# Moving the mask block and the small statistics inside one SBUF arena, and an earlier wait for the load of the spatial bias

## The reference, cut to what matters

```python
# attention, 8 heads of 64, window of 128 keys and 4 sink keys
scores = scale * q @ k.T;  scores = where(keep, scores, -1e9)
a = exp(scores - max(scores));  x = (a / (sum(a) + 1e-9)) @ v
# gated mixer
h = relu(x @ w_in);  u, v = h[..., :512], h[..., 512:]
v_n = (v - mean(v)) / sqrt(var(v) + 1e-6)
v_s = einsum('ts,bsd->btd', w_spatial, v_n) + b_spatial[None, :, None]
y = (u * v_s) @ w_out
# token mixer and channel mixer
h = relu(y.transpose(0, 2, 1) @ w_tok1) @ w_tok2
u = y + h.transpose(0, 2, 1)
out = u + relu(u @ w_ch1) @ w_ch2
```

## Time and profile before

| | us |
|---|---|
| three runs | 523.14, 522.19, 522.09 |
| median | 522.19 |
| the profiled execution, its own time | 523.14 |
| its span on the profile | 521.4 |
| PE busy | 498.1 (96% of the span) |
| DVE, ACT, POOL busy | 217.3, 151.7, 178.5 |

### The profile page before, as it was taken

The page is one execution under the profiler, slowest core; times in us unless marked ns, Lnnn a source line. Parts: engine busy times, 40 slices in busy tenths (PEclk is TensorE's granted clock), DMA queues, the critical chain, the costliest instruction groups (busy, mean ns, idle before and its releaser), DMA issues.

```text
span 521.4 us, 7223 instructions
## 1 busy us (share of the span) xinstructions
PE 498.1 (96%) x2712; PEld 442.9 (85%) x2712; DVE 217.3 (42%) x535; ACT 151.7 (29%) x315; POOL 178.5 (34%) x192
## 2 busy tenths in 40 slices
PE   2589999999999999999999999999999999999997
PEld 1578899999999989999888899888888888888885
DVE  4577777587567434755221232112121121211212
ACT  3246656466555342111221122110101101001010
POOL 5566645375343278900406912950000000000000
PEclk9999999999999999999999999999999999999999
DMA  7524332433220134300201410410001000010002
GB/s 264 163 89 156 104 96 77 126 119 105 84 82 0 47 121 127 92 15 1 75 1 61 137 47 6 136 40 1 0 19 63 0 1 0 18 64 1 0 1 80
DMA packets 19478, 34.18 MB, mean 66 GB/s; under 512 B 2288, under 2 KB 4848, under 8 KB 19440
## 3 DMA queue, kind: packets, MB, share of 16 engines
q1 hardware_dynamic: 19008, 33.55, 20.3%
q10 hardware_dynamic: 432, 0.13, 0.1%
HBM read 30.53 MB, written 3.15 MB: 65 GB/s over the span
## 4 chain that ended last, share of the span: by engine, by line
PE 89%; DVE 4%; issue 2%; DMA 1%; POOL 1%; ACT 1%; DVEq 0%; ACTq 0%; SPq 0%
PE bank L933 23%; PE bank L935 23%; PE bank L934 23%; PE bank L1006 7%; PE bank L972 3%; PE bank L948 2%; PE bank L949 2%; PE bank L1014 1%; PE bank L988 1%; PE bank L1166 1%; DVE q_st L751 1%; DMA mask_scratch<-key 1%; PE bank L1164 1%; DVE masked L760 1%; DMA stage<-w_sp 1%
## 5 line engine op out<-in xcount | busy, mean ns | idle before, releaser
L922 DVE SCALAR_TENSOR_TENSOR hch_lo<-bank,hch_hi 128x512 fp32r<-128x512 f32 x36 | 24.9, 692 | 153.8 <-ACT hch_hi L696 153.8
L696 ACT ACTIVATE hch_hi<-bank 128x512 fp32r<-128x512 f32 x36 | 21.5, 598 | 169.0 <-PE bank L935 169.0
L588 ACT ACTIVATE probs<-masked,small 128x288 f32<-128x288 f32 (+1 forms) x96 | 49.1, 512 | 64.4 <-DVE small L760 64.2
L760 DVE CUSTOM_DVE_ANT_0 masked<-bank,masks 128x288 f32<-128x288 f32 (+1 forms) x96 | 40.9, 427 | 38.4 <-PE bank L949 32.7
L935 PE MATMUL bank<-up_hi,wc_lo 128*128 128x512 f32 x144 | 56.0, 389 | 0.0
L934 PE MATMUL bank<-up_lo,wc_hi 128*128 128x512 f32 x144 | 56.0, 389 | 0.0
L933 PE MATMUL bank<-hch_hi,wc_hi 128*128 128x512 f32 x144 | 56.0, 389 | 0.0
L934 PE MATMUL bank<-hch_lo,wc_hi 128*128 128x512 f32 x144 | 56.0, 389 | 0.0
L933 PE MATMUL bank<-up_hi,wc_hi 128*128 128x512 f32 x144 | 56.0, 389 | 0.0
L935 PE MATMUL bank<-hch_hi,wc_lo 128*128 128x512 f32 x144 | 56.0, 389 | 0.0
L948 PE MATMUL bank<-k_hi,q_st 128*128 128x288 f32 (+1 forms) x96 | 35.5, 372 | 18.2 <-DVE q_st L751 12.8
(11 more groups left out here) (120 smaller groups left out, 1067.2 us busy)
## 6 DMA issues: line engine op xcount, KB each, us to landing
k_raw<-kT SPq DMA_DIRECT2D x24, 256.0 KB, 3.1
q_raw<-qT SPq DMA_DIRECT2D x24, 256.0 KB, 2.7
stage<-w_c SPq DMA_DIRECT2D x24, 256.0 KB, 2.6
v_sl<-vL SPq DMA_DIRECT2D x12, 264.0 KB, 2.8
outT<-out_sb SPq DMA_DIRECT2D x12, 256.0 KB, 2.1
stage<-w_sp SPq DMA_DIRECT2D x12, 192.0 KB, 2.5
stage<-w_in SPq DMA_DIRECT2D x8, 256.0 KB, 3.6
stage<-w_out SPq DMA_DIRECT2D x4, 256.0 KB, 3.2
```

The source lines that it names most:

```text
L588: act.activation(probs[:, n % N_PROB, 0:w], masked[:, n % N_MASKED, 0:w], ACT.Exp, bias=least[:, n % 8:n % 8 + 1], scale=-1.0).then_inc(ex ...
L696: act.activation(hch_hi[:, u[2] % N_HCH, :], bank[:, :], ACT.Relu).then_inc(hi_ready, 1)
L760: dve.tensor_tensor_reduce(masked[:, n % N_MASKED, 0:w], score_bank[n % 2][:, 0:w], masks[:, m:m + w], 1.0, 3e38, ALU.add, ALU.min, least[ ...
L922: dve.scalar_tensor_tensor(out=hch_lo[:, f % N_HCH, :], in0=bank[:, :], scalar=0.0, in1=hch_hi[:, f % N_HCH, :], op0=ALU.max, op1=ALU.subt ...
```

## The change

The order inside the arena changes and one wait is replaced. The masks move from the front part of region A to its end, the small statistics to the end of the arena; `brow` now lies over the masks, 64 columns in, and so it needs the last masked head and no longer the last `x_lo`. Everything from `A_MASKED` to `A_X` starts 1,088 columns lower, everything from `B_X` to `E_IDR` 96 columns lower. An assertion that named offsets are multiples of 128 columns goes.

```diff
 A_VS = A_V + 3 * H * DV
-A_MASKS = A_VS + 2 * GV
-E_SMALL = A_MASKS + MASK_COLS
-A_MASKED = E_SMALL + 96
+A_MASKED = A_VS + 2 * GV
 A_PROBS = A_MASKED + N_MASKED * BAND
 ...
 A_X = A_CAT + P
-A_END = A_X + 2 * DM
+A_MASKS = A_X + 2 * DM
+A_END = A_MASKS + MASK_COLS
 B_X = A_END
 ...
 E_IDR = E_ID + P
-COLS = E_IDR + P
-
-assert all(at % P == 0 for at in (A_V, A_PROBS, A_PT, A_PTS, A_CAT, A_X, B_X, X_SLOT, B_WIN, C_VN, D_U, E_V, E_STAGE, E_ID))
+E_SMALL = E_IDR + P
+COLS = E_SMALL + 96
 ...
-A_BROW = A_CAT
+A_BROW = A_MASKS + 64
 ...
             for n in range(EARLY, EARLY + 3):
                 stage_in(n)
-            sp.wait_ge(x_lo_ready, TILES)
+            sp.wait_ge(masked_ready, N_HEAD)
             sp.dma_start(brow[:, :], b_sp).then_inc(s_brow, 16)
             for n in range(EARLY + 3, len(pieces)):
                 stage_in(n)
```

## The result

| | before | after |
|---|---|---|
| median of 6 runs each, us | 522.64 | 529.58 |
| lowest to highest | 522.09 to 523.81 | 527.68 to 531.05 |
| ratio after / before, 95% interval | | 1.0124 [1.0102, 1.0146] |
| profiled execution, span | 521.4 | 526.5 |

The change makes the kernel 1.2% slower, 5.3 to 7.6 us by the interval. The forecast was no change, at most 523.3. A ratio in this text is the one on record and not always the quotient of two medians: that of the change follows from the median of all 23 recorded runs of the changed kernel, 529.11 us.

A forecast was written before the change was run, and what follows sets the result against it. The prediction took PE as the bound, busy 498.1 of 521.4 us. Its three terms, 0 + 0 + 0, left the earlier median of 522.19 unchanged: 522.1 us, range 521.1 to 523.3.

The forecast's parts named there:

- Part 1, the wait: SP's bias load before the spatial products: goes out about 11.0 us earlier, but PE gains 0, lower end -0.31 us.
- rival (a): Entry to spatial products: PE does wait for the twelfth vn_lo, gain 0.31 us, total 521.9; chance 0.08.
- Part 2, the offsets: Operands of all engines at moved start addresses: no instruction gets longer or shorter, 0 us.
- So PE and DVE pay 0 here: PE products and DVE operations: durations at the four distances in the earlier trace look alike, so moved places cost 0.
- Part 3, transfers: Loads and stores touching moved rows: 0 us, with -0.1 and +0.1 as ends for the last store.
- (b): Start, DVE against POOL at L734: the race turns, DVE gains 1.02 us, total 521.2 or lower; chance 0.10.
- (c): Start, DVE mask chain L717 to L723: late index table loses a race with POOL, 1.1 to 1.4 us, 523.4; chance 0.10.

The follow-up runs named there:

- e5: The changed kernel with the old wait (12 times x_lo) put back, so only the places differ from the kernel before; 529.17 us, ratio 1.0115.
- e3: The kernel before with every buffer, region A too, 32 columns (128 bytes) higher; 523.05 us, ratio 1.0007.
- e2: The kernel before with B_X starting 32 columns (128 bytes) behind A_END, the assertion taken out; 530.41 us, ratio 1.0164.
- e4: The kernel before with 32 columns put in ahead of C_VN only, moving vn, y, w_c2 and the hidden layer; 525.42 us, ratio 1.0037.
- f1: The kernel before with `up` and `hch` products alternating in the mixer, B_X up 32 columns and D_U another 32; 526.96 us, ratio 1.0106.
- f0: The kernel before with `up` and `hch` products alternating one by one in the channel mixer, offsets unchanged; 522.46 us, ratio 0.9998.
- e9: The changed kernel with A_END rounded up by 32 columns; 522.14 us, ratio 0.9997.
- e7: The kernel before with 16 columns (64 bytes) put in ahead of B_X; 525.82 us, ratio 1.0064.
- e10: The kernel before with 48 columns (192 bytes) put in ahead of B_X; 528.2 us, ratio 1.0078.

## Why the prediction was wrong

**Part 1, the wait: right.** Its value was forecast as 0, and no run shows another: e1 (early wait, old offsets) gives 1.0019 [0.9999, 1.004], and e5 (late wait, new offsets) is as slow as the change. The steps came out as worked: bias load at 171.29 (said: near 172), the last vn_lo ahead of everything PE asks for (193.08; said 193.8), PE's start still 0.36 us behind ACT. The reading of vn_ready's value against the named releaser held, and rival (a) fell, most plainly by e5, where PE starts before the twelfth vn_lo has ended. The worked size, at most 0.31 us, was never paid out, since ACT's end decides in both kernels.

**Part 2, the offsets: wrong, and the step that failed is "So PE and DVE pay 0 here".** It put at 0 a term that the stages measure at 5.8 us. The sentence behind it dismissed "-1 and +1 cycle per product" as inside the rounding. What was measured is 5.5 ns for a product of 512 columns in w_out (226.9 to 232.4) and 2.7 ns for one of 384 (173.6 to 176.3), and 1,368 products stand in the four stages that grew. Three things were wrong in that step. First the variable: I compared an operand's place with a fixed grid. e3 shows that the place alone is of no account; e2 and e4 show that the distance between the operands counts. Second the resolution: the earlier trace rows has 10 ns steps (0.30 us), and an effect of 5 ns can't be seen in them. The earlier trace rows has single ns, but the length of a weight load is nearly blind to this effect: for the `up` products, which lose 6 ns each, its minimum, median and maximum are 187/188/188 before and 187/188/193 after. The view of one line has three digits, and it would have shown that the streams of 512 columns behind the attention are even to 3 ns (387/389/390, 389/389/389), a rhythm that had something to lose. Third the place: heads 92 and 93 in the earlier trace rows do happen to have distances 0 and 128 between q and k_lo, but they lie in the interleaved stage, where one such product stands between others. That no rhythm can build up there is my reading; the second token products of e4 and f1, which keep their length at distance 128 among short products, fit it. In the uniform stages, where PE has no slack at all, every product had distance 0. What never varies in the stretch at stake can't be bounded from another stretch, and the range should have carried the end instead of leaving it out.

**Part 3, transfers: about right, and small.** Stores land in 2.0 us in the median against 2.1. That fits in sign what the prediction took from the Trainium skill, page "DMA: Bandwidth & Descriptors", section "How a descriptor splits into AXI transactions". The other runs agree: the six profiles whose rows of `out_sb` start on a multiple of 256 bytes all show 2.0, and of the eight others seven show 2.1 and one (f0) 2.0. The staging loads of w_sp show nothing of the kind: 2.4 against 2.5 here, but 2.6 in e2, e3 and e5, which are aligned, and 2.4 in e1 and e9, which are not. None of it reached PE.

**The rivals on the start.** DVE's mask chain and the races with POOL, after:

```profile
7.15 0.35 DVE L719 SCALAR_TENSOR_TENSOR mask_scratch<-mask_scratch,small 128x128 f32<-128x128 f32 x1
7.53 1.24 DVE L721 TENSOR_TENSOR mask_scratch<-mask_scratch 128x128 f32<-128x128 f32 x1
8.80 0.31 DVE L706 TENSOR_SCALAR masks<-mask_scratch 128x128 f32<-128x128 f32 x1
...
15.29 1.39 DVE L732 TENSOR_TENSOR mask_scratch<-mask_scratch 128x128 f32<-128x128 f32 x1
```

The first race turned for the better (0.35 us for 1.43 in the earlier trace rows) and the one behind it for the worse (1.24 for 0.37); the third stayed lost. The first mask is ready 0.20 us earlier (8.80 + 0.31 = 9.11 against 8.59 + 0.72 = 9.31 before, by this line of the kernel before).

```profile
8.59 0.72 DVE L708 TENSOR_SCALAR masks<-mask_scratch 128x128 f32<-128x128 f32 x1
```

So (b) and (c) describe something real, but it is scatter between executions. e5 differs from the changed kernel only in SP's wait near 170 us, and yet its first race is lost again (1.35 us) and the second won (0.29). The kernel before and f0 are the same program up to the channel mixer, and the first spatial product starts at 195.3 us in one and 193.3 in the other; over the fourteen profiles it is anywhere from 193.3 to 198.1. So nothing here ascribes to the change the 0.7 us by which the changed kernel entered earlier. Rival (c), the slower one, named the wrong place: no rival priced PE's own stream.

**The size.** The sum over the stages, 5.8 us, lies inside the interval of the ratio (5.3 to 7.6 us). For e2 the interval is 6.6 to 10.6 us, and the same stages explain 5.8 of it; for e7 it is 2.0 to 4.7 us, and they explain 1.9. The rest is not explained; a later entry into the spatial products, which scatters, may be part of it.

## What to carry to other kernels

Where PE streams product after product without a hole, keep the start addresses of stationary and moving operand a multiple of 256 bytes apart, from one product to the next as well (e4's switches); when a layout is repacked, round each region's end, even if the assertion that says so looks like tidiness. Read the spread of a group's durations (387/389/390 against 390/394/405) and not only its mean, and multiply nanoseconds by the number of products before calling them rounding. A releaser named by a view is the last engine to touch a semaphore; the value in the code decides whether it was waited for.

## What the runs showed of the hardware

- The rate of back-to-back float32r products depends on the distance between their operands in SBUF: at 0 and 256 bytes starts lie 226 to 227 ns apart in the mean for 512 columns, at 128 bytes 233.0 ns in the mean of the `up` products. Single distances then run from 223 to 242 ns in the changed kernel's mixer.
- The distance has a sign. Moving minus stationary start, modulo 256 bytes, 64 bytes cost a product of 512 columns 2.0 to 2.4 ns and 192 bytes 6.4 to 6.6, in three stages each (e7, e10); a product of 384 columns lost nothing at either and 2.7 ns at 128.
- The loss lasts longer than the mismatch: seven of twelve products of distance 0 were slow behind a group at 128 bytes (231.1 ns, then 226.7 again), and in e4 one product on each side of a switch.
- It was not seen where products of 384 columns stand among short ones of 128: 26.5 (e4) and 26.4 us (f1) against 26.6.
- The effect is reproducible: the mixer lasted 195.2 us in all six profiles with distance 0 or 256, and 199.1 or 199.2 in the three with 128.
- PE's two reads of SBUF are not indifferent to each other's addresses: e3 is e2 with region A moved by the same 128 bytes, and its mixer lasts 195.2 us against 199.2. The Trainium skill, page "SBUF — State Buffer", section "Who interferes with whom", lists two independent read ports of PE, one for the moving operand and one for the weights. These runs don't contradict separate ports, but where the two operands start costs time all the same, and here the measurement decides.
- Why 256 bytes, and which of the simultaneous reads collide, stays open.
